# Order of four steps' work on ScalarE and TensorE in a scan kernel: logarithms earlier, decays before the row copies, next-chunk products before key-value products

## What is computed

```python
mag = np.sqrt(a_re * a_re + a_im * a_im)
scale = np.minimum(mag, 0.999) / (mag + 1e-06)
a_re_n, a_im_n = (a_re * scale, a_im * scale)
for t in range(S):
    ar, ai = (a_re_n[:, :, t, :, None], a_im_n[:, :, t, :, None])
    new_re = ar * S_re - ai * S_im
    new_im = ar * S_im + ai * S_re
    kv = np.einsum('bhd,bhe->bhde', k[:, :, t], v[:, :, t])
    S_re, S_im = (new_re + kv, new_im)
    y[:, :, t] = np.einsum('bhd,bhde->bhe', q[:, :, t], S_re)
```

## Time and profile before

| what | value |
| --- | --- |
| profiled execution, span | 1164.59 us, 1162.8 us |
| attention, from the first transposes to the last copy | 49.6 to 499.4 us |
| PE busy, whole span | 1013.4 us (87%) |
| DVE, ACT, POOL busy, whole span | 645.1, 565.0, 209.3 us |
| TensorE clock granted in the attention | 0.78 of full speed |

### The profile page before, as it was taken

The page is one execution under the profiler, slowest core; times in us unless marked ns, Lnnn a source line. Parts: engine busy times, 40 slices in busy tenths (PEclk is TensorE's granted clock), DMA queues, the critical chain, the costliest instruction groups (busy, mean ns, idle before and its releaser), DMA issues. The chain is left out here.

```text
span 1162.8 us, 27871 instructions
## 1 busy us (share of the span) xinstructions
PE 1013.4 (87%) x10432; PEld 871.0 (75%) x10433; DVE 645.1 (55%) x1369; ACT 565.0 (49%) x911; POOL 209.3 (18%) x193
## 2 busy tenths in 40 slices
PE   0787887887887898747999999999989999999997
PEld 0456655765665666636999999999968888888886
DVE  4388887787787788853555555566552212221210
ACT  6487676767775785412454555544442122222221
POOL 2132121212121212122111110000002222222222
PEclk9677877687787788956999999999989999999999
DMA  9304341433242311084223303312000000000000
GB/s 186 66 18 95 66 94 38 97 76 72 50 97 50 84 39 40 24 288 158 86 66 129 129 21 122 109 29 80 1 1 14 15 28 1 28 1 28 14 14 28
DMA packets 172060, 74.99 MB, mean 64 GB/s; under 512 B 152864, under 2 KB 165280, under 8 KB 171936
## 3 DMA queue, kind: packets, MB, share of 16 engines
q1 hardware_dynamic: 165408, 59.15, 20.3%
q0 software_dynamic: 3072, 9.44, 2.4%
q10 hardware_dynamic: 3456, 4.72, 1.1%
HBM read 63.86 MB, written 9.44 MB: 63 GB/s over the span
## 5 line engine op out<-in xcount | busy, mean ns | idle before, releaser
L1170 PE MATMUL B<-xT,W 128*128 x1488 | 173.5, 277 | 1.3 <-ACT xT L976 1.3
L1170 PEld LDWEIGHTS B<-xT,W 128*128 128x128 f32 x1488 | 171.2, 194 | 2.0 <-issue 2.0
L1099 DVE TENSOR_TENSOR W2l<-W,W2h 128x768 fp32r<-128x768 f32 x124 | 113.2, 955 | 38.0 <-ACT W2h L996 37.5
L1355 PE MATMUL L<-zT,high 128*128 128x512 f32 x324 | 127.3, 393 | 2.2 <-DVE zT_low L1314 2.2
L1355 PE MATMUL L<-zT,low 128*128 128x512 f32 x324 | 127.1, 392 | 0.0
L1355 PE MATMUL L<-zT_low,high 128*128 128x512 f32 x324 | 127.1, 392 | 0.0
L996 ACT ACTIVATE W2h<-W 128x768 fp32r x124 | 104.5, 846 | 34.4 <-PE B L1188 31.6
L298 POOL TENSOR_TENSOR qn<-qe,trig 128x384 f32<-128x384 f32 x48 | 62.8, 1308 | 266.3 <-ACT trig L370 262.9
L1257 POOL TENSOR_TENSOR h_low<-h_full,hz 128x512 fp32r<-128x512 f32 x36 | 46.4, 1289 | 316.8 <-ACT hz L1292 316.8
L1327 DVE TENSOR_TENSOR m<-L,m 128x512 f32<-128x512 f32 x36 | 24.9, 691 | 132.2 <-PE L L1355 132.2
L1292 ACT ACTIVATE hz<-h_full 128x512 fp32r<-128x512 f32 x36 | 22.8, 632 | 151.5 <-DVE h_full L1333 151.5
(11 more groups left out here) (171 smaller groups left out, 2031.6 us busy)
## 6 DMA issues: line engine op xcount, KB each, us to landing
W<-in_moe_w SPq DMA_DIRECT2D x16, 1536.0 KB, 10.6
are<-in_a_re SPq DMA_DIRECT2D x12, 384.0 KB, 3.8
aim<-in_a_im SPq DMA_DIRECT2D x12, 384.0 KB, 5.0
qin<-in_q SPq DMA_DIRECT2D x24, 192.0 KB, 3.2
kin<-in_k SPq DMA_DIRECT2D x24, 192.0 KB, 3.5
vin<-in_v SPq DMA_DIRECT2D x24, 192.0 KB, 2.9
vblk<-in_v SPq DMA_DIRECT2D x96, 48.0 KB, 2.3
attention_rows<-ysb ACTq DMA_DIRECT2D x24, 192.0 KB, 2.8
```

The lines of the kernel that those rows point to most:

```text
L1099: nc.vector.tensor_tensor(W2l[:, g], w2raw[:, bass.ds(base + g * GC, GC)], W2h[:, g], ALU.subtract).then_inc(s["w2_low_ok"], 1)
L1170: ins = nc.tensor.matmul(banks[2 * p + half][:, j % 4 * P:(j % 4 + 1) * P], W1[:, w, c * FF + j * P:c * FF + (j + 1) * P], xf[:, bass.ds(x ...
L1355: ins = nc.tensor.matmul(out_, stationary(a_, c), moving(b_, c), start=(c == 0 and k == 0), stop=(c == count - 1 and k == 2))
```

## The change

The functions that do the work are the same, and so are their numbers; `step` on ACT and on PE calls them in another order. One call, `onward_out(0, 1)`, moves from step 0 into the prologue.

```diff
--- before.py
+++ after.py
@@ -424,44 +424,40 @@
                 batch = batch_at(i, g, more) if n < NG else None
                 hf = half_at(i, g, more) if n < NG else None
                 stage = hf[2] if hf else None
+                if stage == 2:
+                    seed_turn(*hf[:2])
                 if n < NG:
                     turned_q(i, g)
                     turned_k(i, g)
                 if g % 2 == 1:
+                    if batch:
+                        decays(*batch)
                     if n >= 5 and (n - 5) // 2 < NT:
                         wait(act, s["xt_ok"], rows_before(i, g, 1))
                         wait(act, s["lg_ok"], rows_before(i, g, -1))
                         nc.scalar.activation(xT[:, ((g - 1) // 2) % 2], PH[:, 0:DM], ACT.Copy).then_inc(s["xt_out"], 1)
-                    if stage == 2:
-                        logs(*hf[:2])
-                    if stage == 0:
-                        if batch:
-                            decays(*batch)
-                        squares(*hf[:2])
-                        absolute(*hf[:2])
-                    if n >= 3 and n - 3 < NG:
-                        y_rows(i, g)
-                    if stage == 2:
-                        seed_turn(*hf[:2])
-                    if batch and stage != 0:
-                        decays(*batch)
                 else:
                     if batch:
-                        onward_out(*batch)
                         rounded(*batch)
-                    if n >= 3 and n - 3 < NG:
-                        y_rows(i, g)
-                    if batch:
                         steps_out(*batch)
                     if stage == 1:
                         magnitude(*hf[:2])
-                    if batch:
-                        cos_sin(*batch)
-                    if stage == 3:
-                        angle(*hf[:2])
-                    if n >= 6 and (n - 6) // 2 < NT:
-                        wait(act, s["lg_ok"], rows_before(i, g - 1, 1))
-                        nc.scalar.activation(lg[:, bass.ds(i * B + (g - 6) // 2, 1), :], PH[:, 0:2 * E], ACT.Copy).then_inc(s["lg_out"], 1)
+                if n >= 3 and n - 3 < NG:
+                    y_rows(i, g)
+                if stage == 0:
+                    squares(*hf[:2])
+                    absolute(*hf[:2])
+                if g % 2 == 0 and batch:
+                    cos_sin(*batch)
+                if stage == 3:
+                    angle(*hf[:2])
+                if g % 2 == 0 and n >= 6 and (n - 6) // 2 < NT:
+                    wait(act, s["lg_ok"], rows_before(i, g - 1, 1))
+                    nc.scalar.activation(lg[:, bass.ds(i * B + (g - 6) // 2, 1), :], PH[:, 0:2 * E], ACT.Copy).then_inc(s["lg_out"], 1)
+                if stage == 1:
+                    logs(*hf[:2])
+                if g % 2 == 1 and batch:
+                    onward_out(*batch)
 
             act.wait_ge(s["zeroed"], 8)
             squares(0, 0)
@@ -481,6 +477,7 @@
             steps_out(0, 0)
             cos_sin(0, 0)
             decays(0, 1)
+            onward_out(0, 1)
 
             def tile(i, more, static):
                 for g in range(GROUPS):
@@ -829,27 +826,24 @@
                 if prep:
                     turned(i, g, "q")
                     turned(i, g, "k")
+                if batch:
+                    (near if odd else factors)(*batch)
+                if live:
+                    score(i, g)
                 rows = odd and n >= 5 and (n - 5) // 2 < NT
                 if rows:
                     gate_rows(i, g)
-                if batch and odd:
-                    near(*batch)
-                if live:
-                    score(i, g)
                 if n >= 3 and n - 3 < NG:
                     values(i, g)
                 if batch and odd:
                     if rows:
                         wait(pe, s["xt_out"], rows_before(i, g, 1))
                     phases(*batch)
-                if batch and not odd:
-                    factors(*batch)
+                    onward(*batch)
                 if not odd and n >= 6 and (n - 6) // 2 < NT:
                     logits(i, g)
                 if live:
                     key_values(i, g)
-                if batch and odd:
-                    onward(*batch)
 
             pe.wait_ge(s["cst_in"], 48)
             pe.wait_ge(s["zeroed"], 8)
```

## The result

The changed kernel is slower: 1201.49 us median of 4 runs (1198.68 to 1205.38) against 1165.63 us (1163.82 to 1167.85) for the kernel before; the ratio is 1.0309, with a 95% interval of 1.0269 to 1.0349. The forecast was slower, 1194 us, between 1166 and 1208. The profiled execution took 1194.79 us, with a span of 1193.0 us. It is the shortest of the changed kernel's five, so the traces show 30.2 us of difference where the medians show 36. A run more than 1.5% above the fastest of its kernel is left out of that kernel's ratio, which happened only to four of the twelve runs of experiment 9.

What follows compares the result with a forecast made beforehand. Attention paced by a cycle of waits through ACT, PE and DVE, no engine full: 37.0 us a half tile becomes 39.9. Nine times 2.9, less 1, plus 4.5 for jumps, is +29.5 on 1164.59: 1194 us, range 1166 to 1208.

Steps and rivals of the forecast that it cites:

- The cycle: Attention, half tile of four steps: waits through ACT, PE and DVE set the pace, 37.0 us without PE's loop jump.
- QT(S2) to TQ(S3): S2: PE's products into PH, LX and KV all follow xT; 8.4 us, bounds 6.3 and 9.7.
- QT(S1) to QT(S2): S1 on ACT: the logarithms and exponential now stand ahead of QT(S2); 13.8 us where it was 8.4.
- The 3.4 us: PE's row behind xT in S2: the clock comes back about 3.4 us after its start, inside the row.
- TQ(S3) to QT(S1): S3 and S0, DVE and ACT in turn: 17.7 us against 19.4, 1.7 us won.
- a half tile: Four steps of the attention: 39.9 us against 37.0, so +2.9 us, counted nine times.
- The jump: PE's loop jumping back, three times: +1.5 us each, 4.5 in all, bounds 0 and 3 each.
- The first half tile: First S2 with logarithms has no xT, so its products into PH don't wait: about -1 us.
- my sign for it: Whole attention: PE's granted clock falls below 0.78.
- Rival 1: Faster: DVE's lost 3.3 us decide if QT(S2) to TQ(S3) is below 5.5 us; 1137 us, halfway 1150; chance 0.10.
- Rival 2: The clock holds, so S2's row runs at full clock: +7, 1172 us; chance 0.15.
- rival 3: Clock low through S2 into S3; S0's products into PH at half clock end behind the state; +46, 1210 us; chance 0.20.

Runs made afterwards that it cites:

- experiment 9: Also written combo_nofill: changed kernel with key-value products ahead of the products into PH in S2 and ysb behind the sines in even steps; 1177.9 us, ratio 1.0082.
- 1: Changed kernel with the key-value products ahead of the three products into PH again in S2; 1185.11 us, ratio 1.0151 to the kernel before.
- 5: Kernel before with only the logarithms moved to the end of S1 and the exponential to the head of S2; 1202.43 us, ratio 1.0299.
- ysb_late: Changed kernel with the copy of output rows and its store behind the sines and arctangent in even steps; 1193.13 us, ratio 1.0228.
- Run 6: Changed kernel with three more PE products in the idle time ahead of the products into PH in S2, nothing moved; 1180.23 us, ratio 1.0113.
- Combo: Changed kernel with early key-value products in S2, ysb behind the sines in even steps and three added products in S2; 1151.99 us, ratio 0.9875.
- run 2: Changed kernel with xT copied ahead of the decays again on ACT in odd steps; 1200.92 us, ratio 1.0287.

## Why the prediction was right

**The cycle.** The forecast followed one cycle through ACT, PE and DVE, and each link of it is in the new trace: the wait of DVE for `seed_turn` went, PE's row waits for xT, DVE waits for KV, `signed` for the arctangent. That the row behind xT is the cause is shown by step 3, where there is no xT and QT(S2) to TQ(S3) takes 3.6 us, by 1 (a part of it taken out: 16 us) and by 5 (the logarithms alone put it there: the whole loss). The direction and the place were right for the reason given. That the sum came out to 1 us was in part luck, as the terms show.

**QT(S1) to QT(S2).** Forecast 13.8 us, measured 13.76, in every half tile to 0.05 us. ACT works here almost without a gap, and sums of durations hold where one engine is hardly ever waiting.

**QT(S2) to TQ(S3).** Forecast 8.4 us between 6.3 and 9.7, measured 9.0 on average without a jump. Three of these five half tiles stand at the upper end (9.8 us), two at 7.7 and 8.0. I let the clock come back 3.4 us after the row's start, inside it; in six of the eight half tiles KV, the last of the row, still ran at half clock (1.60 us), and behind step 19's row it was 9.1 us from the row's start until the clock came back. The 3.4 us were a misreading: they are the length of the stretch 277.6 to 281 of the earlier trace rows and not the time until the clock rose. In the kernel before, the clock was at 0.50 already ahead of both rows that I took it from, and in step 24 it stayed there for 4.2 us of work:

```profile
56.00:60.30 4.30, 3.20 (x40) 1.89 (x38) 1.17 (x2) 4.25 (x8) 1.86 (x2) 0.50 0.01 4
...
275.10:277.60 2.50, 0.00 (x0) 0.00 (x0) 1.29 (x2) 0.00 (x0) 0.00 (x0) 0.50 0.01 3
277.60:281.80 4.20, 4.14 (x105) 3.52 (x105) 3.18 (x9) 2.03 (x4) 0.00 (x0) 0.50 0.03 10
```

**TQ(S3) to QT(S1).** Forecast 17.7 us, measured 18.8. Nearly all of the 1.1 us is one term: `cos_sin` starts 5.7 us after TQ(S3) on average and not 4.7 (4.7 in two half tiles, 5.45 in step 20, up to 7.6). It stands behind ysb, which waits for the output rows, and in step 20 the transposes ahead of these still ran at half clock. As a difference it was -1.7 against -1.2: the kernel before takes 20.0 us on average where the one half tile I had read took 19.4.

**Repeats and ends.** Without the jumps a half tile grew by 3.8 us (37.8 to 41.6 us, the sums of the table's means), and not by 2.9; over the eight half tiles after step 8 that is 7 us too little. The jump costs 3.1 us before and 3.2 after, so my +1.5 for each of three was 4 us too much. The first half tile, without an xT, was put at -1 us, and TQ of step 4 comes at 79.67 us against 83.25 before. These 3.6 us are not firm: in the trace of ysb_late, with the logarithms in the same place, it comes at 83.66. The half tile from step 4 to step 8 lost 2.7 us. Together the profiled difference of 30.2 us met 29.5 because 7 us too little stand against 4 and 2.6 us too much. Against the medians of the timed runs, 36 us apart, the forecast is 6 us short.

**The clock.** PE stood still from 236.4 us, its clock was at 1.00 for the first 4.1 us and at 0.51 in the last 1.1, and all of the row ran at 0.50. The rule of the Trainium skill (TensorE: Matmul & The Clock Gate, the section on why it matters for kernels), that idle gaps between bursts put the array back to its lower clock, agrees with this. Run 6 shows its price, 21 us. What was wrong is my sign for it in the whole attention: I said the granted clock would fall below 0.78, and it stayed at 0.78. Part of the reason is that the mean counts the idle time, most of it at 1.00. The other is that the half clock moved more than it grew: six rows at 7.5 and not 4.0 us are 21 us more of PE's busy time, and in the whole attention it grew by 9.9, so other work ran faster than before. The mean of a long stretch says little of the clock at which the work that decides ran.

**The rivals.** Rival 1's turning point was 5.5 us from QT(S2) to TQ(S3). With the measured means of the other pieces it is 5.2 (37.8 less 18.8 and 13.8). Combo has 5.45 us there and is faster than the kernel before, but no test of that point, since its other pieces are shorter too (17.6 for 18.8, and 0.9 for a jump and not 3.2). Rival 2 (the clock holds) would have given 1172; with the clock held by added work in S2 it was 1180. Of rival 3, 1210 us, the first half came true in most half tiles, the clock low through S2 into S3; the second did not: in S0 the products into PH ran at full clock, and KV waited up to 1.1 us for the state. Its price, 9 x 4.2, held only S2's row. The median, 1201.5, lies about as near to it as to my 1194.

**Left open.** Why a timed run of the changed kernel lies anywhere between 1195 and 1205 us, and combo_nofill between 1167 and 1187, was not tested. The half tiles of one trace differ by when the clock comes back (TQ(S3) to QT(S1) from 17.8 to 20.7 us), which would give such a spread. Why the jump back costs 3.1 us in one order and 0.9 in another was not tested either.

## What to carry to other kernels

Before work is moved ahead of a wait on one engine, look at what the engine behind it feeds: here the logarithms removed a wait of 3.3 us on DVE and pushed one copy (xT) back by 6 us (from 9.3 us after QT(S1) in step 23 of the kernel before to 15.5), and everything that stood behind that copy in PE's list lost its cover. A piece in which one engine never waits can be summed to 0.05 us; a row that follows an idle time of TensorE like this one (5.3 us) should be priced at half clock to its end, since that was the case in six of eight half tiles. And two lists that were written for each other should be tested in halves only to find mechanisms: each half alone was slower than the whole.

## What was not expected of the hardware

Adding 30 products of 512 columns (2.84 us for three) to an engine that stood still made the kernel 21 us faster in one order and 24 to 26 us in another; the clock of the attention rose from 0.78 to 0.89 in combo. The clock's fall can also make a gain in one place vanish in the next: in run 2, 0.75 us won in S2 went together with a longer idle time in S0 and half-clock transposes behind it.
